# Attention, a routed two-layer expert stage and a feed-forward stage on one core: the experts go one at a time on 128 tokens, with weights and tokens split into a rounded part and a rest

## The reference

```python
# 1: attention, 8 heads of 64, each query sees at most the 128 last keys
scores = np.where(mask, scale * q @ k.T + bias, -1e9)      # q, k, v: (4, 8, 576, 64)
x = softmax(scores) @ v                                    # to (2304, 512)
# 2: routed experts, only tokens with x @ w_skip > 0
e_idx = np.argmax(xc @ w_gate, axis=1)                     # 8 experts
for e in range(8):
    h = np.maximum(xc[mask_e] @ w1[e], 0.0)                # 512 -> 1024
    y[mask_e] = gate_w[mask_e, None] * (h @ w2[e])         # 1024 -> 512
out[do_compute] = xc + y
# 3: feed-forward on all tokens
g = h * np.tanh(softplus(h)), h = out @ w_in               # 512 -> 2048
return g @ w_out                                           # 2048 -> 512
```

## Time and profile before

| what | us |
|---|---|
| median of 3 runs | 783.05 |
| the profiled execution, its own time | 783.5 |
| its span, first to last instruction | 781.7 |
| attention, to the last turn of its result | 0 to 168.3 |
| router, to the first product of the experts | 168.3 to 192.07 |
| expert stage, to the last scaling | 192.07 to 351.8 |
| hand-over | 351.8 to 362.2 |
| feed-forward stage | 362.2 to the end |

### The profile page before, as it was taken

One profiled execution on the slowest core, in us unless ns is written; L12 is line 12 of the kernel. 1 busy time (PEld: TensorE's weight loads), 2 busy tenths in 40 slices (PEclk: granted clock), 3 DMA queues, 4 the chain that ended last, 5 costly groups with the idle time before them and its releaser, 6 DMA issues.

```text
span 781.7 us, 13724 instructions
## 1 busy us (share of the span) xinstructions
PE 764.8 (98%) x4652; PEld 586.8 (75%) x4652; DVE 516.5 (66%) x1138; ACT 366.2 (47%) x885; POOL 109.4 (14%) x254
## 2 busy tenths in 40 slices
PE   8999999998999999999999999999999999999998
PEld 5788888876333333338889989898989898989886
DVE  4667676774111111337998888888878888888885
ACT  5677777730111011442655545464555455545544
POOL 3555555511111020000000000000000000000000
PEclk8999999998999999999999999999999999999999
DMA  6666898612978185004001101010110001001001
GB/s 224 196 182 205 273 285 285 211 31 49 339 288 310 37 303 204 8 16 140 1 2 41 41 0 42 1 41 2 40 41 0 27 14 40 0 0 41 1 1 41
DMA packets 53052, 78.22 MB, mean 100 GB/s; under 512 B 24548, under 2 KB 26212, under 8 KB 52961
## 3 DMA queue, kind: packets, MB, share of 16 engines
q1 hardware_dynamic: 50944, 72.02, 28.1%
q0 software_dynamic: 1600, 4.85, 1.7%
q10 hardware_dynamic: 432, 0.41, 0.2%
HBM read 65.53 MB, written 12.56 MB: 100 GB/s over the span
## 4 chain that ended last, share of the span: by engine, by line
PE 87%; DVE 4%; DMA 3%; issue 2%; ACT 2%; POOLq 0%; POOL 0%; ACTq 0%; SPq 0%; DVEq 0%
PE ps_y L1433 16%; PE ps_xt L1416 12%; PE ps_ht L1416 12%; PE ps_y L1123 9%; PE ps_h L1433 8%; PE ps_h L1105 8%; PE ps_out_t L578 5%; PE ps_probs_t L561 5%; PE ps_scores L550 4%; PE ps_x L589 4%; PE ps_scores L534 2%; DMA x_in<-tokens,job_entry 1%; PE ps_h L1402 1%; DVE h_sb L1015 1%; DMA k_raw<-in_kT 1%
## 5 line engine op out<-in xcount | busy, mean ns | idle before, releaser
L1305 ACT ACTIVATE u_sb<-u_sb 128x384 f32<-128x384 f32 x96 | 50.6, 527 | 105.3 <-DVE u_sb L1353 105.3
L1309 ACT ACTIVATE r_sb<-n_sb,all_consts 128x384 f32<-128x384 f32 x96 | 59.3, 617 | 85.3 <-DVE n_sb L1369 85.3
L382 ACT ACTIVATE probs<-ps_scores,neg_max 128x256 f32<-128x256 f32 (+2 forms) x160 | 66.5, 426 | 30.0 <-DVE neg_max L434 30.0
L1433 PE MATMUL ps_y<-ffn_lo,g_hi 128*128 128x512 f32 x192 | 76.6, 399 | 0.0
L1433 PE MATMUL ps_y<-ffn_hi,g_lo 128*128 128x512 f32 x192 | 75.9, 396 | 0.0
L1433 PE MATMUL ps_y<-ffn_hi,g_hi 128*128 128x512 f32 x192 | 75.7, 395 | 0.0
L434 DVE TENSOR_REDUCE neg_max<-ps_scores 128x1 f32<-128x256 f32 (+2 forms) x160 | 48.6, 362 | 31.7 <-PE ps_scores L550 31.5
L1416 PE MATMUL ps_xt<-xt_hi,ffn_lo 128*128 128x384 f32 x192 | 66.1, 344 | 0.8 <-DVE xt_lo L1344 0.8
L1381 DVE SCALAR_TENSOR_TENSOR u_sb<-n_sb,r_sb 128x384 f32<-128x384 f32 x96 | 53.7, 559 | 19.1 <-ACT r_sb L1311 19.1
L1416 PE MATMUL ps_ht<-xt_hi,ffn_lo 128*128 128x384 f32 x192 | 66.0, 344 | 0.0
L1416 PE MATMUL ps_xt<-xt_hi,ffn_hi 128*128 128x384 f32 x192 | 64.9, 338 | 0.0
(11 more groups left out here) (179 smaller groups left out, 1633.1 us busy)
## 6 DMA issues: line engine op xcount, KB each, us to landing
experts_even<-in_w SPq DMA_DIRECT2D x8, 2048.0 KB, 10.9
w_sb<-in_w SPq DMA_DIRECT2D x8, 2048.0 KB, 12.2
ffn_raw<-in_w_ffn SPq DMA_DIRECT2D x16, 512.0 KB, 5.7
q_raw<-in_qT SPq DMA_DIRECT2D x15, 288.0 KB, 3.9
k_raw<-in_kT SPq DMA_DIRECT2D x15, 288.0 KB, 4.5
v_sb<-in_v SPq DMA_DIRECT2D x16, 256.0 KB, 2.7
tokens<-x_out SPq DMA_DIRECT2D x64, 64.0 KB, 3.7
x_sb<-tokens SPq DMA_DIRECT2D x5, 768.0 KB, 4.5
```

The costliest lines, as they stand in the source:

```text
L382: nc.scalar.activation(probs[0:n, r, h, 0:w], ps_scores[t.ring][0:n, h, 0:w], ACT.Exp, bias=neg_max[0:n, r, h:h + 1], scale=-1.0, accum_ou ...
L1305: nc.scalar.activation(u_sb[:, t.r], u_sb[:, t.r], ACT.Exp).then_inc(u_ready, 1)
L1309: nc.scalar.activation(r_sb[:, t.r], n_sb[:, t.f % NB], ACT.Ln, bias=cst["two"]).then_inc(ln_ready, 1)
L1433: m = nc.tensor.matmul(ps_o[i][:, :], a[:, t.r, P * i:P * i + P], ffn[b][:, at:at + D], start=(t.f == 0 and n == 0), stop=(t.f == FT - 1 a ...
```

## The change

Now an expert is a phase of its own (`PH = E`), and a job is 128 tokens of that one expert (`W = P`). With these tokens experts 2 to 5 need 2 jobs and the others 1: 12 jobs. Weights and tokens of the expert stage are split into `hi` and `lo` as in the feed-forward stage, and each product is three one-pass products. In the first layer the weights are now the stationary operand, 128 columns at a time, and the 128 tokens the moving one, so that the hidden values come out turned already, and `transpose_h` is gone. ScalarE takes the positive part and rounds in one step (`high_h`), VectorE makes its rest (`low_h`).

All weights, experts' and feed-forward's, go through one ring of 22 pieces of 128 x 1024 values; a layer is 8 pieces, and there are 10 layers. SP loads two pieces at a time (`load_part`). During a first job of phase p, ScalarE and VectorE split the 8 pieces of phase p + 1 between their other work; GpSimd makes `lo` of five pieces during the router and of the last four at the end.

```diff
-W = P // 2
-PH = E // 2
+W = P
+PH = E
...
         def hidden(p, i, c):
...
-            for k in range(KD):
-                for side in range(2):
-                    mine = slice(W * side, W * side + W)
-                    m = t_.matmul(ps_h[c][mine, :], x[:, k, mine], weights(p, 0, side, k * F1 + c * half),
-                                  start=(k == 0), stop=(k == KD - 1))
+            for f in range(KD):
+                n = 8 * p + 2 * c + f // 2
+                if first and f % 2 == 0:
+                    lo_wait(pe, cst, n)
+                for k in range(KD):
+                    for step, (a, b) in enumerate((("lo", 0), ("hi", 1), ("hi", 0))):
+                        m = t_.matmul(ps_h[c][:, f, :], ring.at(a, n, f % 2 * half + k * P, P), x[b][:, k, :],
+                                      start=(k == 0 and step == 0), stop=(k == KD - 1 and step == 2))
             m.then_inc(h_ready[p], 1)
...
         def output(p, i, slot, c):
...
             for k in range(KD):
-                for side in range(2):
-                    mine = slice(W * side, W * side + W)
-                    m = t_.matmul(ps_y[slot][mine, :], (h_t, h_t2)[c][:, k, mine],
-                                  weights(p, 1, side, (KD * c + k) * D),
-                                  start=(c == 0 and k == 0), stop=(c == 1 and k == KD - 1))
+                n = 8 * p + 4 + 2 * c + k // 2
+                if isinstance(i, int) and i == 0 and k % 2 == 0:
+                    lo_wait(pe, cst, n)
+                for step, (a, b) in enumerate(((1, "hi"), (0, "lo"), (0, "hi"))):
+                    m = t_.matmul(ps_y[slot][:, :], h_t[c][a][:, k, :], ring.at(b, n, k % 2 * half, half),
+                                  start=(c == 0 and k == 0 and step == 0), stop=(c == 1 and k == KD - 1 and step == 2))
...
             hidden(p, i, 0)
             hidden(p, i, 1)
-            transpose_h(p, i, 0)
-            transpose_h(p, i, 1)
...
# scalar block
+        def high_h(p, i, c):
+            act.wait_ge(h_ready[p], of_all(totals, p, i) * 2 + c + 1)
+            nc.scalar.activation(h_t[c][0][:], ps_h[c][:], ACT.Relu).then_inc(h_hi_ready[p], 1)
+        def one(p, i, slot, total):
+            pieces = [n for n in pieces_of(p, i) if n >= len(HI_ORDER)]
+            high_parts(pieces[0:2])
+            high_h(p, i, 0)
+            high_parts(pieces[2:4])
+            high_h(p, i, 1)
+            high_parts(pieces[4:6])
...
+            high_parts(pieces[6:])
...
# sync block
+        for p in range(PH):
+            done = of_all(totals, p, totals[p])
+            sp.wait_ge(h_ready[p], done * 2)
             settled(sp, cst)
+            load(p + 2, (3,))
+            if p < PH - 1:
+                load(p + 3, (0,))
+                sp.wait_ge(y_ready[p], done)
+                settled(sp, cst)
+                load(p + 3, (1, 2))
```

More of the change, by code:

```diff
@@ L88, in keep_warm @@
         nc.tensor.matmul(bank[:, 0:FILL], cst["ident"], cst["all"][:, 0:FILL], start=True, stop=True)
[L91 to L100, removed]
+HI_ORDER = [3, 4, 5, 6, 7, 0, 1, 2] + list(range(8, 16))
@@ new lines, with hi_count, lo_count, lo_wait @@
+POOL_FIRST = [3, 4, 5, 6, 7]
+POOL_LAST = [76, 77, 78, 79]
+BY_POOL = POOL_FIRST + POOL_LAST
+BY_VECTOR = [n for n in range(8 * LAYERS) if n not in BY_POOL]
+def hi_count(n):
+    return HI_ORDER.index(n) + 1 if n < len(HI_ORDER) else n + 1
+def lo_count(n):
+    return BY_VECTOR.index(n) + 1
+def lo_wait(eng, cst, n):
+    if n in BY_POOL:
+        eng.wait_ge(cst["w_lo_by_pool"], BY_POOL.index(n) + 1)
+    else:
+        eng.wait_ge(cst["w_lo_ready"], lo_count(n))
+def load_part(sp, dram, cst, layer, part):
+    n = 8 * layer + 2 * part
+    sp.dma_start(cst["ring"].raw(n, 2), dram["parts"][4 * layer + part]).then_inc(
+        cst["part_loaded"][layer % 3][part], 16)
@@ L657, in experts @@
     top, chosen, expsum = scratch(TT), scratch(TT), scratch(TT)
-    rank, row, number, job1, side = (scratch(TT) for _ in range(5))
+    rank, row, number, job1 = (scratch(TT) for _ in range(4))
     shifted = by_tile(E)
@@ L772, in _, with load @@
     def _(sp):
-        def load_experts(p):
-            for i, (to, of) in enumerate(pair_weights(dram, pairs[p % 2], p)):
-                if i == 2:
-                    sp.wait_ge(w1_loaded[p], 32)
-                sp.dma_start(to, of).then_inc(w1_loaded[p] if i < 2 else w2_loaded[p], 16)
+        def load(layer, parts):
+            for part in parts:
+                load_part(sp, dram, cst, layer, part)
         sp.wait_ge(weight_spread, 1)
@@ L1085, in transpose_x @@
             m.then_inc(xt_ready[p], 1)
-        def weights(p, layer, side, at):
-            start = (2 * layer + side) * KD * F1 + at
-            return pairs[p % 2][:, start:start + half]
         def hidden(p, i, c):
             x = x_t
-            if isinstance(i, int) and i == 0:
+            first = isinstance(i, int) and i == 0
+            if first:
                 x = x_first
                 if c == 0:
-                    pe.wait_ge(first_copied, p + 1)
-                    pe.wait_ge(w1_loaded[p], 32)
+                    pe.wait_ge(first_lo, p + 1)
@@ L1494, in program @@
             with ExitStack() as buffers:
[L1495 to L1496 removed]
+                wait_stored, wait_bias = attention(nc, part, buffers, block, dram, ffn, cst)
+            own = experts(nc, part, block, wait_stored, wait_bias, dram, ffn, cst)
             feed_forward(nc, part, block, own, dram, ffn, cst, out)
```

400 lines of the change are left out of this document (205 added, 195 removed).

## The result

The changed kernel took **938.68 us**, the median of 4 runs (932.97 to 943.0), against 782.54 us (781.55 to 784.24) for the kernel before on the same chip. The ratio is 1.199, with a 95% interval of 1.191 to 1.207. The forecast was 826 us with a range of 812 to 852: the direction was right, the size was off by 113 us. The profiled execution took 933.0 us, its span is 931.1 us, against 781.7. The runs of experiments 2, 4, 7 and 8 lie 2 to 3% apart, the longer ones with the lower mean clock; ratios are of the faster runs alone, and the profiles are of runs of 952.05, 900.62, 891.62 and 921.6 us.

What follows compares the result with a forecast made beforehand. TensorE, busy 98% of the span, was taken to bound the kernel. 783.5 us plus 40.7 for the expert stage and 2.5 for its start gave 826.7, 826 us as median, with a range of 812 to 852.

Steps and rivals of the forecast that it cites:

- that the clock stays up in the first layer: Expert stage: the first layer's 96 short products run at 2.4 GHz throughout, 10.56 us a job.
- the second rival: Expert stage: the clock falls to 1.2 GHz for half of each first layer, 84 us more, 910 us; chance 0.08.
- The pauses between experts: Expert stage: stalls of TensorE from splits, transfers or gathers, 0 to 2 us a phase, taken as none.
- The start of the stage: Ahead of the first expert product: more register reads and splits, a quicker table; start at 194.6 instead of 192.07, +2.5 us.
- 0 to 3 us, and I take 0: Router: GpSimd's five splits might slow VectorE's small steps beside them by 0 to 3 us; taken as 0.
- The hand-over: Expert stage to feed-forward: chain kept, last splits lie beside it; 0, the rest together between -1 and +2 us.
- Twelve jobs: Expert stage: by the reference's token counts, 10 jobs become 12 when each holds 128 tokens of one expert.
- A product of the first layer at 110 ns: Expert stage: loading 128 stationary columns sets the pace, 110 ns a product; 96 take 10.56 us against 6.89 before.
- The rule of the Trainium skill: Expert stage's first layer: load and product pairs at about 81 ns, giving 793 us; a rival with chance 0.04.
- The second layer at 233 ns: Expert stage: 24 products with 512 moving columns at 233 ns, 5.60 us a job against 7.16 before.
- No wait between the layers: Expert stage: the 0.70 + 0.66 us between a job's layers vanish, as hidden values come out turned.
- Feed-forward and attention unchanged: Both stages keep their products and TensorE waits for no transfers there; 0, the rest together between -1 and +2 us.

Runs made afterwards that it cites:

- experiment 2: The changed kernel, with each second job's first layer also waiting for the scaling of the first job, which puts a pause there; 944.87 us, ratio 1.195.
- experiment 4: The changed kernel with all splits of weights on VectorE and none on GpSimd; 916.31 us.
- experiment 7: The changed kernel without GpSimd's splits, plus five unneeded `keep_warm` products behind the pause at the start of each expert's first job; 887.7 us, ratio 1.121.
- experiment 8: The changed kernel plus five unneeded `keep_warm` products behind each job's last product, ahead of the pause; 919.79 us.
- experiment 3: The changed kernel with each first-layer product running over its 128 tokens twice, 256 moving columns, the second half unused; 865.82 us, ratio 1.106.
- experiment 1: The changed kernel with the job counts of these inputs written into TensorE's program, so without jumps between experts; 846.36 us, ratio 1.080.
- experiment 6: The changed kernel with job counts in TensorE's program, no splits on GpSimd, and 14 unneeded products filling TensorE's wait before the first layer; 827.22 us, ratio 1.055.
- experiment 5: The changed kernel with job counts written into TensorE's program and all GpSimd splits moved to VectorE; 836.44 us, ratio 1.069.

## Why the prediction was wrong

The failed step is one, and it was named: **that the clock stays up in the first layer.** It was the second rival, priced at 910 us, with a chance of 0.08. The argument against it was that the table's slow products came after idle time, and that attention, with short products, keeps a mean clock of 0.98. The first half was a warning read as an excuse: the new stage has idle time in front of a first layer too, eight times. The second half compared unlike things: attention's pairs have 192 or 256 moving columns, and experiment 3 shows that with 256 a fall lasts 3.1 to 6.2 us where with 128 it lasts 15 to 20. The rival's size was low as well: it had half a first layer at half clock, in twelve jobs; it was nearly the whole of it (15.3 to 20.5 us low) in eight, and none in four. 69 + 13.5 = 82.5 us, by luck close to its 84.

**The pauses between experts** were set at 0 to 2 us a phase, with 0 taken. They were 12.9 us in all, in that bound; but what they were bounded by, splits, transfers and gathers, was not their cause. It was the fetching of TensorE's own program, eight times unrolled behind jumps, and no step of the prediction looked at its length. Their larger price is the clock: experiment 1 gives 92 us for both together.

**The start of the stage**: +9.3 and not +2.5 us. The term "0 to 3 us, and I take 0" for GpSimd's five splits was mis-sized: it is 9.0 us (experiment 4). Without them the first product starts at 192.4, where the sum had 194.6: the router began 1.3 us earlier (169.0 instead of 170.3), its table came 0.3 us sooner than priced, and VectorE's register loads took 4.9 us and not 5.6. **The hand-over**, "0, between -1 and +2", was +6.4 us: the budget put four splits of VectorE's beside a chain of transfers, at 1.15 us each. There were six behind the last scaling, two of them from the last job, at 2.59 us each with GpSimd's beside them, and they became the chain. Even without GpSimd's the hand-over was 2.3 us longer than before (experiment 4).

**What was right.** Twelve jobs. A product of the first layer at 110 ns: 111 measured, bounded by rows at 40 and 192 moving columns. One leg of that bound is weaker than it looked. It halved the table's 219 ns, taken at 1.2 GHz; in the changed kernel the table's products (line 1164, with 26 columns) ran at a granted clock of 1.00 and started 132 and 203 ns apart in turn, 159 on the mean, and not 110. Why is open. So the 111 was met partly by luck, and that the weight load sets the pace is the likely reading of these rows, not shown by an experiment. The rule of the Trainium skill (TensorE: Matmul & The Clock Gate, section "Back-to-back issue gap") of about 81 ns for 128 moving columns does not hold for float32r here. The second layer at 233 ns: 2.80 us for 12. No wait between the layers. Feed-forward and attention unchanged, within 2.6 us. Experiment 6, which has the changed kernel's products without the pauses and without GpSimd's splits (it has the job counts in TensorE's program, gives the splits to VectorE and adds 14 calls of `keep_warm` ahead of the stage), takes 827.2 us with a stage of 200.5 us: the sum of 826.7 was the price of the products, and the 111 us above it are what it left out. That the two agree to 1 us is partly chance, since its hand-over is 2 us longer and its start 1 us earlier than in the sum, and since the turns of the next tokens took 0.44 us and not 0.59 while the products took 111 ns and not 110.

Open is what decides a single fall: in experiment 2, behind like pauses of 1.1 to 1.2 us, two first layers fell and two did not.

## What to carry to other kernels

Price a stream of short products at both clocks. Where it stands behind a pause of the engine, even one of a microsecond, half clock was here the likelier case (8 of 8, 6 of 8) and not a rival of 0.08; and read the granted clock by windows, since the busy share shows nothing of it. Count TensorE's own instructions and jumps as a possible wait of their own: fixed job counts were worth 92 us here. Fewer unrolled copies behind the jumps, which would keep the counts free, were not tried. Work given to GpSimd is not free while VectorE has two-operand steps on the path.

## What the runs showed of the hardware

- Float32r products with 128 stationary columns start 111 ns apart with 128 moving columns and 118 ns with 256, at 2.4 GHz; 214 ns with 128 at 1.2 GHz. The record of a weight load is 192 ns long at the one clock and 333 at the other, and overlaps the product before; that it sets the pace is an inference.
- More work was faster: 256 instead of 128 moving columns took 73 us off the kernel. The clock still fell in 4 of 8 first jobs, for 3.1 to 6.2 us of the layer instead of 15.3 to 20.5 in 8 of 8.
- Behind pauses of TensorE of 1.1 to 2.6 us, these layers of 128-column products fell to half clock in 8 of 8 first jobs of the changed kernel, in 6 of 8 without GpSimd's splits, in 2 of 4 second jobs given a pause; without a pause in none of 38 (4 in the changed kernel, 11 each in experiments 1 and 5, 12 in experiment 6).
- One GpSimd subtraction of 128 x 1024 (2.37 us) made VectorE's steps of 0.2 to 0.4 us with two inputs last up to 2.5 us; two such streams side by side ran at 3.3 us a piece each, instead of 1.13 (VectorE) and 2.4 (GpSimd).
- Where TensorE jumped to an expert's code, its next product started 1.50 to 1.67 us after the end of a 16 KB instruction fetch, in seven of seven pauses.
- Straight-line code on TensorE with the same work fetched 0.62 MB of instructions instead of 0.88 and had no pause at all; its four runs lay within 1.7 us, those of the changed kernel within 10.
